# Windowed attention ahead of two MLPs: from 36 slots of four query blocks to 18 slots of eight on 64x64 tiles

## The chip, the cores and the metric

The kernel runs on one core of one Trainium2 chip. The metric is the device time of one execution in microseconds. Three runs of the kernel before took 893.42, 893.79 and 894.28 us, median 893.79.

## What is computed

The input is 4 batches of 8 heads of 576 positions, 64 wide. Each position attends to itself and the 63 before it; the result goes through a gated MLP with RMS norm and through a squared-ReLU MLP. All is fp32.

```python
scores = (q @ k.T) / 8;  mask = (rel >= 0) & (rel < 64)      # rel = query position - key position
scores = where(mask, scores, -1e9);  scores -= scores.max(-1)
attn = exp(scores);  attn = attn / (attn.sum(-1) + 1e-9);  x = attn @ v      # per batch and head
x = x / sqrt(mean(x * x) + 1e-6) * rms_g                      # 2304 tokens x 512
x = (silu(x @ w_gate) * (x @ w_val)) @ w_out                  # d_ff 1536
h = relu(x @ w_in);  out = (h * h) @ w_down                   # d_ff 2048
```

## The kernel before, in words

Channels are on partitions. Two heads of a batch share the 128 partitions, so there are 16 sequences (`SEQS`) of 9 blocks of 64 queries, 144 blocks in all. A block needs the keys of its own 64 positions and of the 64 before. Each of the five engines has its own instruction stream, written out by hand; semaphores join them, and each engine works strictly in the written order.

Attention runs in `GROUPS = 36` groups of four blocks, software-pipelined over slots `g` (0 to 41): in slot g every engine does its part of the group that lags by a constant. TensorE (`slot`, `value_product`) does the scores of group g (L609; 128x128, with the queries of the two heads on the diagonal of a zeroed tile `q_diag`; L604 adds a mask for a sequence's first block), the transposes of group g - 4 (L617, four of `wide`), and in odd slots the value products of two earlier groups (L636, two 128x64 tiles a block). VectorE picks the own keys' columns into place (L1169, `copy_predicated`), takes the maximum (L1178), shifts by it (L1184), and for the group before sums the exponentials (L1175) and inverts (L1181). ScalarE does one Exp per group (L934), copies the transposed weights out of PSUM (L859, `probsT<-bank`) and copies outputs (L859, `acts<-bank`). GpSimd multiplies by the inverse sum (L504) and widens to both key blocks under the mask (L510). Scores, transposes and outputs have two PSUM banks each; banks 0 and 1 are free for the norm.

SP issues all loads in one queue, in the order of the sequences: keys and queries three sequences ahead (a load of keys waits until the sequence whose buffer it takes has its scores), values one ahead (waits on the value products), and between them the first two weight steps (`load_w`) and two chunks of `w_out` (`load_d`).

Tokens are handled in three pairs of 384. The first pair is complete long before the last group, so its squares, norm, splitting into high and low fp32r parts and the first MLP step (`plain(0)`: eight products of six 128x384 matmuls) are spread over slots 16 to 41. Behind the last slot TensorE waits for the last output copy and starts `plain(1)`, then the rest of both MLPs (L661 to L663).

## Time and profile before

| | |
|---|---|
| median of 3 runs | 893.79 us |
| profiled execution | 893.3 us |
| its span, first to last instruction | 891.6 us |
| granted TensorE clock, mean | 1.000 |
| TensorE, VectorE, ScalarE, GpSimd busy | 98%, 63%, 52%, 65% |
| slots of the attention | 0 to 101.7 us |

The profile was taken from one execution. Times are counted from the start of its span. "Busy" is the time between the start and the end of at least one instruction; matmuls overlap, so their mean length (about 0.27 us) says little, and the distance between their starts says more. The fp32 matmuls of the attention show as two MATMUL records each.

### The profile page before, as it was taken

How to read it: one execution, taken by the hardware profiler on the slowest of the kernel's cores; microseconds unless marked ns; L12 is line 12 of the kernel's file. 1: busy time of each engine (PE TensorE's matmuls, PEld its weight loads, DVE VectorE, ACT ScalarE, POOL GpSimd, SP SyncE). 2: the span in 40 equal slices, each digit the busy share in tenths (PEclk: the TensorE clock that was granted, in tenths of full speed). 3: DMA queues.
4: the chain of work that ended last, by engine and by line, in shares of the span. 5: the costliest groups of instructions: out<-in, count | busy, mean ns of one | idle time of the engine just before them, and what ended most of it. 6: DMA issues, size and time to landing. Idle time of an engine off the chain costs nothing.

```text
span 891.6 us, 15074 instructions
## 1 busy us (share of the span) xinstructions
PE 877.7 (98%) x5644; PEld 867.9 (97%) x5644; DVE 561.8 (63%) x735; ACT 463.2 (52%) x800; POOL 575.3 (65%) x539
## 2 busy tenths in 40 slices
PE   7998999999999999999999999999999999999998
PEld 6888999999999999999999999999999999999998
DVE  7778667548657557855556767667377675577222
ACT  3676565644566644455545455554355543455332
POOL 7898479765389757368867368573386653585332
DMA  8996122212222212222221322122422122421122
GB/s 231 263 243 154 53 71 73 71 54 60 79 76 72 68 53 69 73 72 72 71 72 60 82 66 72 54 65 67 148 72 72 54 64 67 148 71 30 49 71 95
DMA packets 105975, 77.00 MB, mean 86 GB/s; under 512 B 24496, under 2 KB 89008, under 8 KB 105904
## 3 DMA queue, kind: packets, MB, share of 16 engines
q1 hardware_dynamic: 105152, 75.60, 30.5%
q8 instruction: 45, 0.74, 0.4%
q10 hardware_dynamic: 752, 0.44, 0.2%
q14 instruction: 26, 0.21, 0.1%
HBM read 71.31 MB, written 4.72 MB: 85 GB/s over the span
## 4 chain that ended last, share of the span: by engine, by line
PE 93%; DMA 3%; DVE 2%; SPq 1%; ACT 0%; issue 0%; POOL 0%; ACTq 0%
PE bank L661 30%; PE bank L662 29%; PE bank L663 29%; DMA q_diag<-in_qT 3%; PE bank L609 2%; PE bank L636 1%; PE bank L617 1%; PE bank L655 0%; PE bank L646 0%; DVE acts L1126 0%; DVE bank L1169 0%; SPq L355 0%; DVE sums L1175 0%; DVE neg_max L1178 0%; DVE probs L1184 0%
## 5 line engine op out<-in xcount | busy, mean ns | idle before, releaser
L661 PE MATMUL bank<-xc_hi,w_hi 128*128 128x384 f32 x844 | 282.8, 335 | 1.7 <-DVE xc_lo L1158 1.0
L663 PE MATMUL bank<-xc_hi,w_lo 128*128 128x384 f32 x844 | 282.0, 334 | 0.0
L662 PE MATMUL bank<-xc_lo,w_hi 128*128 128x384 f32 x844 | 281.9, 334 | 0.0
L552 POOL TENSOR_TENSOR d_lo<-d_raw,d_hi 128x512 fp32r<-128x512 f32 x84 | 127.3, 1516 | 174.5 <-ACT d_hi L859 174.5
L661 PE MATMUL bank<-hs_hi,d_hi 128*128 128x384 f32 x672 | 225.1, 335 | 0.1
L663 PE MATMUL bank<-hs_hi,d_lo 128*128 128x384 f32 x672 | 224.5, 334 | 0.0
L662 PE MATMUL bank<-hs_lo,d_hi 128*128 128x384 f32 x672 | 224.5, 334 | 0.0
L1259 DVE TENSOR_TENSOR hs_lo<-h,hs_hi 128x768 fp32r<-128x768 f32 x84 | 86.4, 1029 | 137.2 <-ACT hs_hi L859 137.0
L661 PEld LDWEIGHTS bank<-xc_hi,w_hi 128*128 128x128 f32 x844 | 158.5, 188 | 2.3 <-DVE xc_lo L1158 1.3
L662 PEld LDWEIGHTS bank<-xc_lo,w_hi 128*128 128x128 f32 x844 | 158.5, 188 | 0.0
L663 PEld LDWEIGHTS bank<-xc_hi,w_lo 128*128 128x128 f32 x844 | 158.4, 188 | 0.0
L859 ACT ACTIVATE hs_hi<-h 128x768 fp32r<-128x768 f32 x84 | 70.9, 843 | 138.7 <-PE bank L663 138.7
L1103 DVE TENSOR_TENSOR w_lo<-w_raw,w_hi 128x1024 fp32r<-128x1024 f32 (+1 forms) x60 | 81.6, 1360 | 82.3 <-ACT w_hi L859 82.2
L661 PEld LDWEIGHTS bank<-hs_hi,d_hi 128*128 128x128 f32 x672 | 126.1, 188 | 1.4 <-issue 0.7
L662 PEld LDWEIGHTS bank<-hs_lo,d_hi 128*128 128x128 f32 x672 | 126.2, 188 | 0.0
L663 PEld LDWEIGHTS bank<-hs_hi,d_lo 128*128 128x128 f32 x672 | 126.2, 188 | 0.0
L859 ACT ACTIVATE w_hi<-w_raw 128x1024 fp32r<-128x1024 f32 (+1 forms) x120 | 111.9, 932 | 0.0
L476 POOL TENSOR_TENSOR w_raw<-w_raw 128x256 f32<-128x256 f32 x58 | 63.7, 1098 | 38.1 <-DMA w_raw<-in_w_val 19.9
L1112 DVE TENSOR_TENSOR w_lo<-w_raw,w_hi 128x768 fp32r<-128x768 f32 (+1 forms) x60 | 72.5, 1209 | 0.0
L545 POOL TENSOR_TENSOR h<-sbb,vb 128x384 f32<-128x384 f32 x34 | 55.7, 1638 | 25.6 <-ACT sbb L983 25.5
L989 ACT ACTIVATE sa<-ga 128x384 f32<-128x384 f32 x58 | 30.5, 526 | 65.9 <-DVE ga L1280 65.8
L859 ACT ACTIVATE c_t<-bank 128x384 f32<-128x384 f32 x58 | 28.5, 492 | 65.3 <-PE bank L663 65.3
(90 smaller groups left out, 1156.0 us busy)
## 6 DMA issues: line engine op xcount, KB each, us to landing
d_raw<-in_w_down SPq DMA_DIRECT2D x48, 256.0 KB, 2.6
w_raw<-in_w_gate SPq DMA_DIRECT2D x36, 256.0 KB, 2.9
w_raw<-in_w_val SPq DMA_DIRECT2D x72, 128.0 KB, 2.9
d_raw<-in_w_out SPq DMA_DIRECT2D x36, 256.0 KB, 2.7
w_raw<-in_w_in SPq DMA_DIRECT2D x24, 256.0 KB, 2.7
w_raw<-in_w_in SPq DMA_DIRECT2D x48, 128.0 KB, 2.6
out_T<-acts SPq DMA_DIRECT2D x24, 192.0 KB, 2.6
k_sb<-in_kT SPq DMA_DIRECT2D x15, 288.0 KB, 4.7
```

The source lines that it names most:

```text
L476: nc.gpsimd.tensor_tensor(raw_part(u, RAW_S3), raw_part(u, RAW_A11), raw_part(u, RAW_A21), ALU.subtract).then_inc(s_add, 1)
L545: nc.gpsimd.tensor_tensor(h_half(n, 1), sbuf_b[:], vb[:], ALU.mult).then_inc(hb_done, 1)
L552: nc.gpsimd.tensor_tensor(d_lo[m % 2][:], d_raw[m % 2][:], d_hi[m % 2][:].bitcast(F32), ALU.subtract).then_inc(dlo_done, 1)
L609: mm = pe.matmul(ps, q_diag[par][:, b, :], keys, start=b > 0, stop=True)
L661: pe.matmul(ps, w_h, v_h, start=first, stop=False, skip_group_check=joined)
L662: pe.matmul(ps, w_h, v_l, start=False, stop=False, skip_group_check=joined)
L663: return pe.matmul(ps, w_l, v_h, start=False, stop=last, skip_group_check=joined)
L859: nc.scalar.activation(to, of, ACT.Copy).then_inc(done, 1)
L989: nc.scalar.activation(sa[:], ga[:], ACT.Silu if first_layer(r) else ACT.Relu).then_inc(act_a_done, 1)
L1103: nc.vector.tensor_tensor(w_lo[u % 2][:, to], w_raw[u % 2][:, of], w_hi[u % 2][:, to].bitcast(F32), ALU.subtract).then_inc(lo1_done, 1)
L1112: nc.vector.tensor_tensor(w_lo[u % 2][:, to], w_raw[u % 2][:, of], w_hi[u % 2][:, to].bitcast(F32), ALU.subtract).then_inc(lo2_done, 1)
L1259: nc.vector.tensor_tensor(hs_lo[m % 2][:], h_chunk(r, m - M0[r]), hs_hi[m % 2][:].bitcast(F32), ALU.subtract).then_inc(hlo_done, 1)
```

## The change

The groups become 18 of eight blocks, four pairs to a group (`UNITS`), in slots 0 to 20. A block's scores are now two 64x64 matmuls, one a head, on four quarters of the array: for blocks 0 to 3 of a group head 0 goes to partitions 0 to 63, for blocks 4 to 7 the heads are crossed. The queries are loaded as they are, without the zeroed tile, the keys in plain order, the values as six blocks per half. Own and previous keys are picked by one mask for all blocks. The maximum is scaled on GpSimd and enters the Exp as its bias; there are eight Exp per group, of 64 columns each, each writing its sum. One transpose takes two blocks. VectorE multiplies the transposed weights by the mask while it takes them out of the single PSUM bank `pt_ps`, once for the own and once for the previous keys; the value products accumulate the two in PSUM. Score banks become two pairs, the outputs share one pair. The norm's banks and slots move (13 to 20), the low halves of the first two weight steps move from VectorE to GpSimd, the order of loads changes.

The diff, cut to what the text speaks of (behind it, `plain(0)` is spread over slots 18 to 20, the squares on ScalarE over slots 7 to 11, `root` in 13, `x_high` in 16 to 20; VectorE normalises in slots 15 to 18 and does `x_low` in 17 to 20):

```diff
 
 SEQS = KT * BATCH
 BLOCKS = SEQS * NBLK
-GU = 4
+UNITS = 4
+GU = 2 * UNITS
 GW = GU * P
 GROUPS = BLOCKS // GU
-S_LAG, N_LAG, T_LAG, PV_LAG, O_LAG = 1, 2, 4, 5, 6
+N_LAG, T_LAG, PV_LAG, O_LAG = 1, 2, 3, 3
 TAIL = GROUPS + O_LAG
-PR = 5
-ER = 3
-QR = 3
+PR = 4
+QR = 4
 VR = 3
 TR = 3
...
+        banks2 = [ctx.enter_context(nc.psum_tensor(f"banks{n}", [P, 1024], F32)) for n in range(4)]
+        bank = [banks2[n // 2][:, n % 2 * 512:(n % 2 + 1) * 512] for n in range(8)]
+        s_ps, pt_ps, o_ps = banks2[0:2], bank[4], banks2[3]
 
...
-                    sp.dma_start(dst[:].rearrange("p m c -> p (m c)"), src[bass.ds(i * P, P), :]).then_inc(v_in[n], 16)
...
+                sp.dma_start(v_sb[n][:].rearrange("p m c -> p (m c)"), v_rows[bass.ds(i * P, P), :]).then_inc(v_in[n], 16)
 
...
             for i in range(SEQS):
+                if i + 1 < SEQS:
+                    load_v(i + 1)
                 if i + QR < SEQS:
                     load_k(i + QR)
                     load_q(i + QR)
-                if i + 1 < SEQS:
-                    load_v(i + 1)
-                if i in (3, 5):
-                    load_w((i - 3) // 2)
-                if i in (8, 9):
-                    load_d(i - 8)
+                if i in (1, 3):
+                    load_w((i - 1) // 2)
+                if i in (9, 10):
+                    load_d(i - 9)
...
+            def low1_plain(u):
+                pool.wait_ge(hi1_done, u + 1)
+                to = slice(0, 3 * HALF_K)
+                nc.gpsimd.tensor_tensor(w_lo[u][:, to], w_raw[u][:, to], w_hi[u][:, to].bitcast(F32),
+                                        ALU.subtract).then_inc(lo1_done, 1)
...
-                    n = g - N_LAG
-                    v = probs[n % PR][:, :, 0:WIN]
+                n = g - N_LAG
+                if 0 <= n < GROUPS:
+                    total = sums[:, n % PR, :]
+                    pool.wait_ge(exp_done, n + 1)
+                    nc.gpsimd.tensor_scalar(total, total, 1e-9, None, ALU.add).then_inc(summed, 1)
+                if g < GROUPS:
+                    peak = neg_max[:, g % PR, :]
+                    pool.wait_ge(maxed, g + 1)
+                    nc.gpsimd.tensor_scalar(peak, peak, SCALE, None, ALU.mult).then_inc(biased, 1)
...
                     pool.wait_ge(inverted, n + 1)
...
+                    nc.gpsimd.tensor_tensor(probs[n % PR][:], probs[n % PR][:],
+                                            by_unit(sums[:, n % PR, :]), ALU.mult).then_inc(scaled, 1)
...
+                if g in (5, 7):
+                    low1_plain((g - 5) // 2)
+                if g in (6, 8):
+                    low2_plain((g - 6) // 2)
+                if g in (9, 10, 11):
+                    add_squares(0, g - 8)
+                if g == 12:
+                    for k in (1, 2, 3):
+                        add_squares(1, k)
+                if g == 14:
...
+            def score(ps, half, seq, b, mask):
+
+                par = seq % QR
+                keys = k_sb[par][:].rearrange("p (n c) -> p n c", c=WIN)
+                for head in range(2):
+                    r = rows(head)
+                    to = ps[rows(head ^ half), :]
+                    if mask:
+                        mm = pe.matmul(to, ident_bf[r, r], first_mask[r, :], start=True, stop=False)
+                    else:
+                        both = keys[r, b - 1:b + 1, :] if b else keys[r, 0:1, :].broadcast_to([WIN, 2, WIN])
+                        mm = pe.matmul(to, q_sb[par][r, b * WIN:(b + 1) * WIN], both, start=b > 0, stop=True)
+                return mm
...
+                        pe.wait_ge(exp_done, g - 1)
+                    for j in range(UNITS):
+                        for half in range(2):
+                            u = half * UNITS + j
+                            seq, b = blocks(g)[u]
+                            ps = s_ps[g % 2][:, u * P:(u + 1) * P]
+                            if b == 0:
+                                score(ps, half, seq, b, True)
+                            mm = score(ps, half, seq, b, False)
...
+                if 0 <= g - PV_LAG < GROUPS:
+                    value_product(g - PV_LAG)
...
+                    pe.wait_ge(scaled, n + 1)
+                    if n >= 1:
+                        pe.wait_ge(pt_out, n)
+                    for j in range(UNITS):
+                        mm = pe.transpose(pt_ps[:, j * P:(j + 1) * P],
+                                          probs[n % PR][:, j, :, :].rearrange("p h c -> p (h c)"), ident[:])
...
+                if n >= 1:
+                    pe.wait_ge(o_out, O_DONE[n])
...
+                for j in range(UNITS):
+                    for own in (1, 0):
+                        for half in range(2):
+                            u = half * UNITS + j
+                            seq, b = blocks(n)[u]
+                            if own or b > 0:
+                                at = (1 - own) * UNITS * P + j * P
+                                v = v_sb[seq % VR][rows(half), held(seq, half).index(b - 1 + own), :]
+                                for head in range(2):
+                                    mm = value(o_ps[rows(head), (UNITS + u) * WIN:(UNITS + u + 1) * WIN],
+                                               v[:, rows(head)],
+                                               probsT[n % TR][rows(half), at:at + P][:, rows(head ^ half)], own, b)
...
+                if g == 17:
+                    pe.wait_ge(exp_done, 17)
+                    spread_half(1, bank[1])
...
+                if g == 13:
+                    token_sums(0, bank[5])
+                if g == 15:
+                    spread_half(0, bank[5])
+                if g == 18:
                     pe.wait_ge(lo1_done, 1)
-                    pe.wait_ge(norm_done, KT)
                     plain(0, "ga", P_A11, "B11")
...
+                    act.wait_ge(biased, g + 1)
+                    if g >= PR:
+                        act.wait_ge(tr_done, g - PR + 1)
+                    for u in range(GU):
+                        mm = nc.scalar.activation(probs[g % PR][:, u % UNITS, u // UNITS, :], s_ps[g % 2][:, u * P:u * P + WIN], ACT.Exp,
+                                                  bias=neg_max[:, g % PR, u:u + 1], scale=SCALE,
+                                                  accum_out=sums[:, g % PR, u:u + 1])
+                    mm.then_inc(exp_done, 1)
...
+                    nc.vector.copy_predicated(
+                        merged, pick[:].unsqueeze(1).broadcast_to([P, GU, WIN]).bitcast(mybir.dt.uint16),
+                        s_view[:, :, 1, :]).then_inc(picked, 1)
                 if g < GROUPS:
+                    if g >= PR:
+                        dve.wait_ge(exp_done, g - PR + 1)
                     dve.wait_ge(picked, g + 1)
-                    nc.vector.tensor_reduce(peak, merged, AX_X, ALU.max, negate=True).then_inc(maxed, 1)
-                if 0 <= g - S_LAG < GROUPS:
-                    dve.wait_ge(summed, g - S_LAG + 1)
-                    nc.vector.reciprocal(total, total).then_inc(inverted, 1)
-                if g < GROUPS:
-                    dve.wait_ge(maxed, g + 1)
-                    nc.vector.tensor_tensor(probs[g % PR][:, :, 0:WIN], merged,
-                                            peak.unsqueeze(2).broadcast_to([P, GU, WIN]), ALU.add).then_inc(shifted, 1)
-
-                if g in (19, 21):
-                    low1((g - 19) // 2)
-                if g in (20, 22):
-                    low2((g - 20) // 2)
-                if g == 28:
-                    mean_square(0, bank[0])
-                if g == 29:
+                    nc.vector.tensor_reduce(neg_max[:, g % PR, :], merged, AX_X, ALU.max,
+                                            negate=True).then_inc(maxed, 1)
+                if 0 <= g - N_LAG < GROUPS:
+                    n = g - N_LAG
+                    dve.wait_ge(summed, n + 1)
+                    nc.vector.reciprocal(sums[:, n % PR, :], sums[:, n % PR, :]).then_inc(inverted, 1)
+                if 0 <= g - T_LAG < GROUPS:
+                    n = g - T_LAG
+                    if n == 0:
+                        dve.wait_ge(consts, CONSTS)
+                    dve.wait_ge(tr_done, n + 1)
+                    if n >= TR:
+                        dve.wait_ge(pv_done, n - TR + 1)
+                    nc.vector.tensor_tensor(
+                        probsT[n % TR][:].rearrange("p (s j q) -> p s j q", s=2, j=UNITS),
+                        pt_ps.rearrange("p (j q) -> p j q", j=UNITS).unsqueeze(1).broadcast_to([P, 2, UNITS, P]),
+                        mask_t[:].rearrange("p s h c -> p s (h c)").unsqueeze(2).broadcast_to([P, 2, UNITS, P]),
+                        ALU.mult).then_inc(pt_out, 1)
```

## Rows read from the trace of the kernel before

**Rows 1.** The page: busy time and share of each engine.

```profile
PE 877.7 (98%) x5644; PEld 867.9 (97%) x5644; DVE 561.8 (63%) x735; ACT 463.2 (52%) x800; POOL 575.3 (65%) x539
```

**Rows 2.** Busy time by engine and stretch, then granted clock, DMA, GB/s.

```profile
12.00:72.00 60.00, 57.67 (x746) 52.31 (x747) 44.66 (x141) 38.84 (x98) 53.38 (x61) 1.00 1.12 256
72.00:101.70 29.70, 26.74 (x318) 24.34 (x316) 22.60 (x48) 19.49 (x44) 24.44 (x25) 1.00 0.36 101
101.70:891.60 789.90, 786.71 (x4548) 785.09 (x4548) 486.72 (x527) 402.75 (x657) 490.42 (x426) 1.00 0.24 71
```

**Rows 3.** Chain that ended last at the hand-over (start, length, what).

```profile
101.12 0.39 ACT acts L859
...
101.77 0.41 PE bank L661
102.18 0.17 PE bank L662
```

**Rows 4.** Timeline of TensorE, one pair of groups (start, length first).

```profile
24.46 1.16 PE L609 MATMUL bank<-k_sb,q_diag 128*128 128x128 f32 x8
25.46 0.60 PE L617 MATMUL bank<-ident,wide 128*128 128x128 f32 x4
...
27.43 0.34 PE L636 MATMUL bank<-probsT,v_even 128*64 128x64 f32 x4
27.59 0.29 PE L636 MATMUL bank<-probsT,v_odd 128*64 128x64 f32 x4
...
28.74 0.38 PE L609 MATMUL bank<-k_sb,q_diag 128*128 128x128 f32 x1
```

**Rows 5.** DMA issues, 12 to 72 us: KB each, us to landing.

```profile
q_diag<-in_qT SPq DMA_DIRECT2D x24, 144.0 KB, 6.4
```

**Rows 6.** Waits before 130 us: total, times, longest.

```profile
DVE bank L1169 <- PE bank L609: 16.2, 16, 2.4
...
PE bank L604 <- DMA q_diag<-in_qT: 6.5, 4, 4.8
```

**Rows 7.** VectorE, groups by line before 130 us (busy, mean ns).

```profile
L1169 DVE COPY_PREDICATED bank<-valid,bank 128x256 f32<-128x256 uint16 x36 | 15.3, 425 | 16.5 <-PE bank L609 16.2
...
L1178 DVE TENSOR_REDUCE neg_max<-bank 128x4 f32<-128x256 f32 x36 | 14.9, 414 | 0.0
L1181 DVE RECIPROCAL sums<-sums 128x4 f32<-128x4 f32 x36 | 6.0, 167 | 0.0
...
L1103 DVE TENSOR_TENSOR w_lo<-w_raw,w_hi 128x1024 fp32r<-128x1024 f32 x4 | 4.9, 1225 | 5.2 <-ACT w_hi L859 5.2
```

**Rows 8.** ScalarE, groups by line before 130 us.

```profile
L859 ACT ACTIVATE probsT<-bank 128x512 f32<-128x512 f32 x36 | 21.3, 592 | 12.1 <-PE bank L617 12.0
L934 ACT ACTIVATE probs<-probs 128x256 f32<-128x256 f32 x36 | 15.0, 417 | 23.5 <-DVE probs L1184 23.2
L859 ACT ACTIVATE acts<-bank 128x256 f32<-128x256 f32 x24 | 8.9, 369 | 1.8 <-PE bank L636 1.8
...
L888 ACT ACTIVATE sq<-acts 128x384 f32<-128x384 f32 x8 | 4.1, 517 | 0.1
...
L934 ACT ACT_TABLE_LOAD x2 | 2.6, 1283 | 2.6 <-issue 2.6
...
L859 ACT ACTIVATE acts<-bank 128x64 f32<-128x64 f32 x8 | 1.7, 211 | 0.0
```

**Rows 9.** Timeline of ScalarE, two output copies of 128 columns.

```profile
27.56 0.42 ACT L859 ACTIVATE acts<-bank 128x128 f32<-128x128 f32 x2
```

**Rows 10.** GpSimd, groups by line before 130 us.

```profile
L510 POOL TENSOR_TENSOR wide<-probs,valid 128x512 f32<-128x512 f32 x36 | 42.9, 1191 | 5.0
L504 POOL TENSOR_TENSOR probs<-probs,sums 128x256 f32<-128x256 f32 x36 | 22.8, 633 | 7.3 <-DVE sums L1181 7.2
...
L466 POOL MEMSET probs<- 128x4 f32 x5 | 0.2, 112 | 0.0
```

**Rows 11.** Timeline of TensorE, the first score passes.

```profile
4.84 4.33 PE L609 MATMUL bank<-k_sb,q_diag 128*128 128x128 f32 x18
```

332 lines of the change are left out of this document (136 added, 196 removed).

## The prediction

> **What bounds the kernel now.** I read the profile page first [rows 1]: TensorE is busy for 98% of the span, no other engine for more than 65%. Then a table of three stretches [rows 2]. The change touches only what lies before 101.7 us. From there to the end TensorE is busy for 786.7 of 789.9 us on code that the change leaves alone, so whatever is won or lost is the moment at which this stretch starts: the matmuls of the second plain step, which now follow the last output copy at 101.77 us [rows 3]. I call that moment H. The profiled execution took 893.3 us, of which 891.6 are its span; the time after is 893.3 - 101.8 + H. (The median of the runs is 893.8, 0.5 above the profiled one; 0.2% of it, 1.8 us, is about what a measurement of this kernel can tell from no change.)
>
> Then the order of work on TensorE in one pair of attention groups [rows 4]: scores from 24.46, transposes from 25.46, again scores and transposes, values from 27.43, and the next scores at 28.74. That is 4.28 us for eight blocks, without a gap, and 18 such pairs make 77 us. The reader should see that every fp32 matmul is two passes: 8 score passes and the change of tile shape behind the values in 1.00 us (0.11 us a pass), 4 transposes in 0.43, 32 value passes in 1.31. Value passes are cheap because two 128x64 tiles run side by side: 4 passes (two matmuls) start every 0.12 us, 29 ns each. The transfers are the second bound: over 12 to 72 us the 16 DMA engines are busy beyond 100% at 256 GB/s [rows 2], with the query tiles landing after 6.4 us in 144 KB pieces of 256-byte runs [rows 5]. TensorE still waited only 6.5 us for them, most of it at the start, and VectorE waited 16.2 us for score matmuls [rows 6], so it has room.
>
> **The change part by part, for one slot of eight blocks.**
>
> *Scores.* The zero-padded query tile goes, and 8 products of 128x128 become 16 of 64x64, 32 passes of 128 columns on four quarter tiles. The trace has no quarter tile. Bounds for a pass: 58 ns if a tile's own cadence (0.12 us for its two passes, [rows 4]) is never overlapped; 15 ns if four tiles overlap as two do now. I take 22, near the low end, because the value passes show that neighbours with different output partitions overlap fully. 32 x 0.022 = 0.70, plus 0.17 for the change of tile shape (the last transpose starts at about 27.23, values at 27.43, against 0.11 within a row of transposes).
>
> *Values.* The 16 matmuls of 64 columns over 128 keys become 32 over 64 keys, less the two that a first block lacks: 60 passes on average. Bounds 15 and 58 ns again; I take 25, since two tiles manage 29 today. 60 x 0.025 = 1.50. This is more than the 1.31 of now.
>
> *Transposes.* 4 in place of 8: 0.44, plus 0.17 for the shape. TensorE then works 0.87 + 1.50 + 0.61 = 3.0 us per slot against 4.28.
>
> *VectorE.* It loses the sum (0.42) and the shift (like 0.42) per four blocks and gains the masked product. From 256 elements in 0.425 and 1024 in 1.225 [rows 7], an element costs 1.04 ns: predicated copy of 512 elements 0.69, maximum 0.68, reciprocal 0.17, product of 1024 elements out of PSUM 1.22. Together 2.8, off the path as a sum.
>
> *ScalarE.* It loses two copies of 0.592 and two Exp of 0.417 [rows 8] and gains eight Exp of 64 columns with a bias from memory and a sum written out. Lower bound 0.09: two 128-column copies take 0.42, so the second adds 0.15, less 0.06 for 64 columns fewer [rows 8, 9]. Upper bound 0.42, the whole Exp of 256 columns. I take 0.33: the 0.21 of a lone 64-column copy plus 0.12 for delivering the sum, as an operation this small cannot cost less than what a second copy adds. 8 x 0.33 + 0.7 for the two output copies = 3.3. Here the Trainium skill bears on one term: "ScalarE: Activation LUTs", section "What ACT_TABLE_LOAD costs", has 280 + 0.833 N ns for a bias from memory and 93 ns of overlap, an estimate of 0.24 for each without the sum; ScalarE would then need 2.6 us a slot and never be late, and H would be some 2 us earlier. No row of this trace shows a bias from memory.
>
> *GpSimd.* Its widening (1.191) and scaling (0.633) per four blocks become one scaling of 512 elements, 1.2 by the row of the widening, and two operations on eight numbers, 0.11 each [rows 10]. 1.4 a slot, so it has room for the low halves of the first two weight steps moved there from VectorE (two of 768 and two of 256 elements, 1.8 and 0.6 each by the widening row) and for the adds.
>
> *DMA.* Queries come as one 288 KB piece like the keys, values as 384 KB in place of 512: 0.98 MB per pair of heads instead of 1.11. At today's 256 GB/s that is 3.8 us per nine blocks, 3.4 a slot, and less if whole rows move faster than 256-byte runs. The first two weight steps and chunks are issued two pairs of heads earlier or one later, each behind the same queue; 1 MB of weights is 4 us of transfer before slot 8, covered while loads run two slots ahead. The value load waits for the product three groups on, and key and query loads queue behind it on SP; they then have some 4.7 us until their slot. I allow 1 us.
>
> *The cycle that sets a slot.* One bank for the transposed tiles closes a ring between two engines: transposes 0.60 from first start to last end, product 1.22, values 1.50, shape 0.17, two hand-overs of 0.05. That is 3.6 us; scores (0.87) fit beside the product. ScalarE's 3.3 lies just under it. So T = 3.6 against 4.28.
>
> *Start and normalisation.* First scores at 4.8 as now. At the start a pass takes twice as long: 18 in 4.33 us, 0.24 each, against 0.111 later [rows 11, 4], though the granted clock reads 1.00 there. Slot 1 needs the second query load, issued only after the first landed: 4.6 + 3.4 = 8.0 (the first loads take 4.0 from their issue to the first score). With half-rate scores and the fill of the ring, slot 3 starts at about 13. Fifteen slots to slot 18: 54 us. Squares (8 x 0.517), the high parts of the weights (two each of 768 and 256 elements, about 0.8 and 0.4) and two table loads (1.283 each) [rows 8] are 9 us on ScalarE, whose slack is 0.3 a slot, 4 in all: +5. In front of slot 17 TensorE waits for the Exp of group 16, so that 1.6 to 3 us, which overlapped before, lie open: +3 with the spread. Slot 18 begins at 75. The tail holds three value groups (4.5), two sets of transposes (1.2), the eight products of the first plain step, six matmuls of 0.18 each [rows 3], 8.6 in all, and 4.5 of waits for products, normalised halves and the last output copy: 18.8. H = 93.8.
>
> **Time: 893.3 - 101.8 + 93.8 = 885.3 us.** Nothing behind H changes: the sums of the third weight step on GpSimd, due about 9 us after H, start with a load issued 15 us before H.
>
> **The rivals.**
> *Quarter tiles overlap fully and Exp is cheap.* Passes of 15 ns and Exp of 0.24 or less: the ring is 3.0, the transfers hold it at about 3.2. Twelve of the 0.4 x 15 saved plus a shorter tail give H near 82: 873.5. For it: two tiles overlap perfectly today. Against: 2 instructions every 15 ns has no row.
> *The Exp with its sum sets the slot (slower).* Place: ScalarE, eight instructions per slot where one or two stood. It decides from 0.38 each on; at 0.42 a slot is 8 x 0.42 + 0.7 + the extra 0.6 = 4.7, H = 106: 897.5. At 0.38 the result is a draw. For it: per-instruction cost, not columns, dominates at 64 columns (0.21 against 0.37 for 256).
> *TensorE falls to half its rate.* Its busy share drops from 96% [rows 2] to some 80% with an idle stretch in each slot while the product runs. Passes twice as long give 5.7 a slot: H near 117, 908.5. Rows 11 show the half rate only behind an idle start, and short waits later never brought it back. The Trainium skill's "TensorE: Matmul & The Clock Gate", section "A second HAM failure mode: psum-queue depth-cycling", names exactly such idling between groups as a cause of falling back from 2.4 to 1.2 GHz; the trace of before neither confirms nor excludes it.
> *Quarter tiles do not overlap.* 58 ns a pass: ring 6.4, H near 140, 931. The change then doesn't do what it says.
>
> **How the numbers follow.** Forecast 885.3 (own range 878 to 893): 0.50. Cheap case: 0.17. A draw with Exp near 0.38: 0.07. Slower by Exp: 0.13. Half rate: 0.08. No overlap: 0.05. Faster 0.49 + 0.16 = 0.65, same 0.09, slower 0.26. For 8 in 10 the range leaves out half rate, no overlap and the far end of the cheap case: 872 to 900.
>
> **What would show it.** The time between score groups should be 3.6 us; value passes 25 ns apart; Exp starts 0.33 apart; the product waiting for transposes and the values for the product in turn; the stretch behind H unchanged at 789.9 us. I am wrong on the ring if TensorE waits for Exp instead; on the quarter tiles if four passes of different tiles start farther than 0.12 us apart; on the clock if the same pass has two lengths in the middle of the attention.

## The result and the profile after

| | before | after |
|---|---|---|
| median | 894.03 us (4 runs, 893.42 to 898.21) | 885.12 us (4 runs, 884.67 to 885.68) |
| ratio after/before, 95% interval | | 0.9891 [0.9860, 0.9921] |
| profiled execution, its span | 893.3, 891.6 | 885.7, 884.0 |
| H, start of the second plain step's matmuls | 101.8 | 94.2 |
| behind H | 789.9 | 789.8 |

The kernel is 1.1% faster, and all of it lies ahead of H. The page of the changed kernel, first its busy times, then TensorE's granted clock in 40 slices (tenths), then the queue of its instruction packets (packets, MB, share of 16 engines):

```profile
PE 858.6 (97%) x6388; PEld 846.9 (96%) x6388; DVE 548.2 (62%) x617; ACT 472.3 (53%) x1000; POOL 543.9 (62%) x517
...
PEclk9998999999999999999999999999999999999999
...
q8 instruction: 51, 0.84, 0.4%
```

TensorE is busy for 19 us less than in [rows 1], in 744 instructions more, yet the span is only 7.6 us shorter: TensorE now stands still for longer ahead of H. Where, is in the busy times by stretch. The stretches are those of the argument: first slots, slots 3 to 6, slots 7 to 12, slots 13 to 16, slot 17 and the tail, and what lies behind H. The columns are busy us (instructions) of TensorE, its weight loads, VectorE, ScalarE, GpSimd, then granted clock, DMA share and GB/s.

```profile
4.80:14.65 9.85, 7.22 (x106) 5.78 (x107) 3.94 (x7) 4.94 (x32) 1.84 (x5) 1.00 0.89 314
14.65:31.80 17.15, 12.75 (x395) 11.18 (x395) 12.31 (x19) 14.28 (x82) 9.46 (x17) 1.00 0.72 222
31.80:52.30 20.50, 17.44 (x594) 14.24 (x594) 14.76 (x23) 19.48 (x107) 13.87 (x23) 1.00 0.87 279
52.30:74.50 22.20, 16.64 (x420) 14.39 (x419) 13.92 (x23) 19.61 (x96) 11.82 (x19) 0.88 0.50 165
74.50:94.20 19.70, 17.84 (x337) 16.31 (x337) 15.98 (x19) 10.03 (x30) 11.65 (x12) 0.88 0.28 76
94.20:884.00 789.80, 786.67 (x4550) 785.01 (x4548) 487.32 (x528) 402.66 (x656) 491.93 (x426) 1.00 0.25 71
```

The last line answers to the last of [rows 2]: 789.8 against 789.9, the same work. In the third line ScalarE is busy for 19.48 of 20.50 us. These are six slots of 3.42 us on average (one by one 2.6, 3.1, 3.6, 4.0, 4.1 and 3.1), and ScalarE is the fullest engine in them; whether it sets them is what the experiments ask. One slot there, first on TensorE, then ScalarE's first Exps of it (start, length, engine, what, count; [idle time <- released by]):

```profile
34.38 1.10 PE L613 MATMUL banks<-k_sb,q_sb 64*64 64x128 f32 x32
35.77 1.15 PE L669 MATMUL banks<-probsT,v_sb 64*64 64x64 f32 x60 [0.28 <-DVE probsT L1224]
36.85 0.66 PE L643 MATMUL banks<-ident,probs 128*128 128x128 f32 x4
```

```profile
34.84 0.31 ACT L976 ACTIVATE probs<-banks,neg_max 128x64 f32<-128x64 f32 x1 [0.24 <-POOL neg_max L519]
35.05 0.19 ACT L976 ACTIVATION_READ_ACCUMULATOR probs<-banks,neg_max 128x1 f32 x1
35.14 0.30 ACT L976 ACTIVATE probs<-banks,neg_max 128x64 f32<-128x64 f32 x1
...
35.43 0.31 ACT L976 ACTIVATE probs<-banks,neg_max 128x64 f32<-128x64 f32 x1
```

An Exp that also writes its sum is two instructions, and the next one starts 0.29 us behind it (34.84, 35.14, 35.43). The 60 value passes, of 1.15 us from first start to last end, start within 0.93 us, 16 ns apart. The groups by line before H (busy us, mean ns | idle us before, releaser) answer to [rows 7, 8, 10]:

```profile
L976 ACT ACTIVATE probs<-banks,neg_max 128x64 f32<-128x64 f32 x144 | 43.1, 344 | 10.2 <-POOL neg_max L519 10.0
L976 ACT ACTIVATION_READ_ACCUMULATOR probs<-banks,neg_max 128x1 f32 x144 | 33.8, 238 | 0.0
...
L1224 DVE TENSOR_TENSOR probsT<-banks,mask_t 128x1024 f32<-128x1024 f32 x18 | 21.6, 1203 | 4.1 <-PE banks L643 4.0
...
L522 POOL TENSOR_TENSOR probs<-probs,sums 128x512 f32<-128x512 f32 x18 | 19.0, 1058 | 1.0 <-DVE sums L1216 1.0
...
L1211 DVE TENSOR_REDUCE neg_max<-banks 128x8 f32<-128x512 f32 x18 | 12.5, 692 | 1.6
L1204 DVE COPY_PREDICATED banks<-pick,banks 128x512 f32<-128x512 uint16 x18 | 12.4, 690 | 20.4 <-PE banks L613 20.4
...
L515 POOL TENSOR_SCALAR sums<-sums 128x8 f32<-128x8 f32 x18 | 4.3, 237 | 21.7 <-ACT probs L976 21.5
```

TensorE's idle time in the two stretches with the lower granted clock (slots 14 and 17):

```profile
56.71 1.50 PE L677 MATMUL banks<-ones,sq 128*128 128x1 f32 x12 [1.00 <-POOL sq L507]
...
59.36 2.07 PE L669 MATMUL banks<-probsT,v_sb 64*64 64x64 f32 x60
...
72.90 1.65 PE L684 MATMUL banks<-sq,ones 128*128 128x128 f32 x6 [3.53 <-ACT probs L976]
74.48 1.99 PE L613 MATMUL banks<-k_sb,q_sb 64*64 64x128 f32 x32
76.24 1.93 PE L669 MATMUL banks<-probsT,v_sb 64*64 64x64 f32 x60
```

The same 32 score passes take 1.99 us here and 1.10 in the slot above, the same 60 value passes 1.93 to 2.07 and 1.15: the same pass has two lengths. The longer one is that of the lower clock level, 1.2 GHz: the granted clock reads 0.50 from 74.5 to 79.2 us, and 0.72 over 72 to 84 us, part at one level and part at the other. In front of each of the two stretches stands a wait of TensorE, of 1.00 and of 3.53 us.

The start of each slot's scores, read off the timelines of this kernel and of those below, is the measure for the rest. The mask products are counted out, and every profile is shifted so that its first matmul stands at 4.84 us as in the changed kernel (by 0.21 us at most; the lines of views are not shifted):

| kernel | slot 3 | 7 | 13 | 14 | 15 | 16 | 17 | H | median us | ratio to before |
|---|---|---|---|---|---|---|---|---|---|---|
| changed | 14.7 | 31.8 | 52.3 | 58.1 | 62.3 | 66.2 | 74.5 | 94.2 | 885.12 | 0.9891 [0.9860, 0.9921] |
| changed, again | 14.6 | 31.2 | 51.9 | 57.8 | 60.4 | 65.7 | 73.2 | 92.4 | 884.39 | 0.9886 [0.9868, 0.9904] |
| no sum | 13.8 | 30.6 | 51.0 | 56.7 | 60.7 | 64.6 | 70.8 | 90.0 | 880.51 | 0.9838 [0.9825, 0.9850] |
| two banks | 14.6 | 31.2 | 51.4 | 57.7 | 60.2 | 65.5 | 73.0 | 91.2 | 888.49 | 0.9922 [0.9897, 0.9947] |
| copies on VectorE | 14.7 | 30.2 | 51.0 | 57.2 | 61.5 | 65.7 | 73.2 | 94.0 | 886.26 | 0.9908 [0.9893, 0.9922] |
| spread in bank 5 | 14.7 | 30.3 | 51.7 | 57.6 | 61.8 | 65.9 | 73.7 | 93.7 | 885.15 | 0.9892 [0.9879, 0.9905] |
| spread behind slot 17 | 14.6 | 31.5 | 52.8 | 58.7 | 62.9 | 67.0 | 70.0 | 89.8 | 880.25 | 0.9834 [0.9816, 0.9852] |
| keys ahead of values | 14.6 | 30.6 | 54.1 | 59.9 | 64.1 | 68.2 | 76.6 | 96.5 | 886.09 | 0.9905 [0.9888, 0.9923] |
| both orders | 14.7 | 28.5 | 52.6 | 58.5 | 62.7 | 66.6 | 69.8 | 89.7 | 881.22 | 0.9839 [0.9821, 0.9858] |
| one half at a time | 16.0 | 34.1 | 62.1 | 67.7 | 72.9 | 77.3 | 84.9 | 109.3 | 892.08 | 0.9981 [0.9961, 1.0000] |
| small loads | 14.6 | 28.0 | 48.7 | 55.0 | 59.8 | 63.7 | 71.2 | 90.8 | 881.50 | 0.9854 [0.9842, 0.9867] |
| token sums behind scores | 14.6 | 30.7 | 51.4 | 55.5 | 60.6 | 65.2 | 68.1 | 87.7 | 878.93 | 0.9826 [0.9813, 0.9839] |
| and early copies on VectorE | 14.6 | 30.6 | 51.9 | 55.1 | 61.3 | 65.8 | 69.0 | 88.8 | 881.53 | 0.9864 [0.9843, 0.9884] |

The kernels ran in three series, on more than one chip, with the kernel before at 895.15, 894.78 and 894.86 us beside them; small differences are read from the ratios, and where their intervals overlap, a difference is not clear of noise. A profile is one execution; between two executions of one kernel slots 4 to 12 shift by up to some 2 us.

### The profile page after: what moved, and what is told of

It reads as the page before. It is cut to its first block, busy times and chain, and to the rows that moved or that the text cites. A ratio compares the mean times of both kernels' runs of the same rounds, so it can differ in the third digit from the quotient of the medians.

```text
span 884.0 us, 16543 instructions
## 1 busy us (share of the span) xinstructions
PE 858.6 (97%) x6388; PEld 846.9 (96%) x6388; DVE 548.2 (62%) x617; ACT 472.3 (53%) x1000; POOL 543.9 (62%) x517
## 4 chain that ended last, share of the span: by engine, by line
PE 93%; ACT 2%; DVE 2%; DMA 1%; issue 1%; POOL 1%; SPq 0%; DVEq 0%; POOLq 0%
PE banks L703 30%; PE banks L705 30%; PE banks L704 30%; ACT probs L976 2%; PE banks L613 1%; PE banks L669 1%; DMA q_sb<-in_qT 1%; DVE probsT L1224 1%; PE banks L684 0%; PE banks L677 0%; PE banks L643 0%; POOL sq L507 0%; DVE neg_max L1211 0%; DVE banks L1204 0%; DVE acts L1164 0%
## 5 line engine op out<-in xcount | busy, mean ns | idle before, releaser
L703 PE MATMUL banks<-xc_hi,w_hi 128*128 128x384 f32 x844 | 282.5, 335 | 0.2 <-DVE xc_lo L1196 0.2
L705 PE MATMUL banks<-xc_hi,w_lo 128*128 128x384 f32 x844 | 281.9, 334 | 0.0
L704 PE MATMUL banks<-xc_lo,w_hi 128*128 128x384 f32 x844 | 281.9, 334 | 0.0
L703 PE MATMUL banks<-hs_hi,d_hi 128*128 128x384 f32 x672 | 225.1, 335 | 0.1
L705 PE MATMUL banks<-hs_hi,d_lo 128*128 128x384 f32 x672 | 224.5, 334 | 0.0
L704 PE MATMUL banks<-hs_lo,d_hi 128*128 128x384 f32 x672 | 224.5, 334 | 0.0
L703 PEld LDWEIGHTS banks<-xc_hi,w_hi 128*128 128x128 f32 x844 | 158.5, 188 | 0.5 <-DVE xc_lo L1196 0.5
L704 PEld LDWEIGHTS banks<-xc_lo,w_hi 128*128 128x128 f32 x844 | 158.5, 188 | 0.0
L705 PEld LDWEIGHTS banks<-xc_hi,w_lo 128*128 128x128 f32 x844 | 158.4, 188 | 0.0
L899 ACT ACTIVATE hs_hi<-h 128x768 fp32r<-128x768 f32 x84 | 70.8, 843 | 138.7 <-PE banks L705 138.7
L704 PEld LDWEIGHTS banks<-hs_lo,d_hi 128*128 128x128 f32 x672 | 126.2, 188 | 0.0
L1030 ACT ACTIVATE sa<-ga 128x384 f32<-128x384 f32 x58 | 30.5, 526 | 65.9 <-DVE ga L1323 65.8
L899 ACT ACTIVATE c_t<-banks 128x384 f32<-128x384 f32 x58 | 28.5, 492 | 65.3 <-PE banks L705 65.3
```

What stands on the lines that cost most here:

```text
L703: pe.matmul(ps, w_h, v_h, start=first, stop=False, skip_group_check=joined)
L704: pe.matmul(ps, w_h, v_l, start=False, stop=False, skip_group_check=joined)
L705: return pe.matmul(ps, w_l, v_h, start=False, stop=last, skip_group_check=joined)
L899: nc.scalar.activation(to, of, ACT.Copy).then_inc(done, 1)
L1030: nc.scalar.activation(sa[:], ga[:], ACT.Silu if first_layer(r) else ACT.Relu).then_inc(act_a_done, 1)
```

## The experiments

The first four part two theories. A: ScalarE with its eight Exps a slot holds the attention. B: the ring transposes, product, values through one bank of transposed tiles holds it.

**No sum.**

```diff
                     for u in range(GU):
                         mm = nc.scalar.activation(probs[...], s_ps[g % 2][...], ACT.Exp,
-                                                  bias=neg_max[:, g % PR, u:u + 1], scale=SCALE,
-                                                  accum_out=sums[:, g % PR, u:u + 1])
+                                                  bias=neg_max[:, g % PR, u:u + 1], scale=SCALE)
```

> The changed kernel without the sum that each Exp writes out (the sums stay at one, so the weights are not normalised; this part is left out). In the changed kernel an Exp and its accumulator read start 0.29 us apart, 0.09 of it behind the read: 144 x 0.09 = 13 us of ScalarE. Theory A (ScalarE sets the slot in the middle of the attention, it is busy 19.5 of 20.5 us there): 4 to 9 us faster than the changed kernel's 885.1. Theory B (the ring transposes, product, values sets it, as predicted): within 1.5 us of it.

Measured 880.51 us, ratio 0.9838, 4.6 us under the 885.12 that the expectation starts from: theory A's range. ScalarE's eight Exps of a slot, in its timeline:

```profile
51.82 1.81 ACT L977 ACTIVATE probs<-banks,neg_max 128x64 f32<-128x64 f32 x8
```

1.81 us against the 2.48 of the changed kernel: 0.21 from start to start in place of 0.29. But slots 7 to 12 still take 3.4 us each (30.6 to 51.0), though ScalarE is no longer full there:

```profile
31.80:52.30 20.50, 17.41 (x596) 14.13 (x590) 15.88 (x25) 17.20 (x66) 14.57 (x25) 1.00 0.87 289
```

Of these six slots four take 3.05 to 3.15 us and two, starting at 39.9 and 43.9, take 4.0; in those two TensorE's values have a gap of 0.96 and 0.98 us in their midst, which the profile puts down to "issue". So where ScalarE has room a slot without a gap takes the ring's 3.05 to 3.15 us, and 2 us are lost to the gaps. The changed kernel has two such long slots too, and slots of 3.1 beside them, so this run alone doesn't say that ScalarE held its middle; the kernel with small loads, below, does. What the lighter Exp won came mostly outside the middle: slots 0 to 2 (0.9 us) and from slot 13 on (51.0 to 90.0, 39.0 us against 40.5 and 41.9 in the two profiles of the changed kernel).

**Two banks for the transposed tiles.**

```diff
-        s_ps, pt_ps, o_ps = banks2[0:2], bank[4], banks2[3]
+        s_ps, o_ps = banks2[0:2], banks2[3]
+        def pt_bank(n):
+            return bank[4 + (n % 2 if n <= 10 else 0)]
...
-                if 0 <= g - PV_LAG < GROUPS:
-                    value_product(g - PV_LAG)
                 if 0 <= g - T_LAG < GROUPS:
                     n = g - T_LAG
+                    pt_ps = pt_bank(n)
                     pe.wait_ge(scaled, n + 1)
-                    if n >= 1:
-                        pe.wait_ge(pt_out, n)
+                    if n >= 2:
+                        pe.wait_ge(pt_out, n - 1 if n <= 10 else n)
...
+                if 0 <= g - PV_LAG < GROUPS:
+                    value_product(g - PV_LAG)
```

> The changed kernel with two PSUM banks for the transposed tiles up to group 10 and the transposes ahead of the values in a slot, so that the product runs beside the values and the ring is open. Theory B: the slot falls from 3.6 towards the 3.1 us of ScalarE in nine slots, 4 to 6 us faster. Theory A: within 1.5 us of 885.1, because ScalarE's work is unchanged.

Measured 888.49 us, between 882.8 and 892.1 in six runs. Neither theory had it slower, and its ratio of 0.9922 [0.9897, 0.9947] overlaps with that of the changed kernel. The 4 to 6 us of theory B are not there: in the profiled execution, the fastest of the six, slots 7 to 12 take 3.37 us each against 3.42. As a limit in slots 3 to 10 the ring falls. Why the other five runs are 4 to 9 us longer, no profile shows; it stays open. Their mean granted clock is 0.992 to 0.996, like that of the changed kernel's runs, and that of the profiled one is 1.000: it ran ahead of H without any stretch at 1.2 GHz, though it has the same wait ahead of the second spread:

```profile
72.29 0.94 PE L688 MATMUL banks<-sq,ones 128*128 128x128 f32 x6 [3.47 <-ACT probs L980]
73.16 1.10 PE L616 MATMUL banks<-k_sb,q_sb 64*64 64x128 f32 x32
```

So a wait of this length doesn't by itself bring the lower clock.

**The output copies on VectorE.**

```diff
 # ScalarE
-                    act.wait_ge(pv_done, n + 1)
-                    for run in runs_of(n):
-                        to, of = output(n, run)
-                        copy(to, of, o_out)
 # VectorE, ahead of the reciprocal
+                    dve.wait_ge(pv_done, n + 1)
+                    for run in runs_of(n):
+                        to, of = output(n, run)
+                        nc.vector.tensor_copy(to, of).then_inc(o_out, 1)
```

> The changed kernel with the output copies (0.7 us a slot) on VectorE in front of the reciprocal, off ScalarE. Theory A: ScalarE has 2.3 us of Exp left a slot, 5 to 9 us faster than 885.1, until VectorE (2.8 + 0.7 = 3.5 a slot) holds it. Theory B: the copies push the product back within the ring, no change to 6 us slower.

Measured 886.26 us, ratio 0.9908: theory A's gain is not there. Busy time over slots 7 to 12, and what TensorE and ScalarE waited for from 24 to 50 us (us in total, times, longest):

```profile
31.80:52.30 20.50, 16.53 (x555) 13.38 (x547) 18.60 (x34) 17.55 (x99) 14.18 (x22) 1.00 0.85 275
```

```profile
ACT probs L970 <- POOL neg_max L519: 4.2, 6, 1.3
PE banks L669 <- DVE probsT L1224: 2.8, 5, 0.9
```

ScalarE went from 19.5 to 17.6 us and VectorE from 14.8 to 18.6: ScalarE now waits for the maximum that VectorE makes later. Over its own slots 7 to 12, 3.47 us each, VectorE is busy for 3.0 us a slot, ScalarE for 3.0, and the ring takes 3.0: none is full. The load moved and nothing was won; that the engines now wait for each other in turn is argued from these waits, not shown.

**The second spread in bank 5.**

```diff
-                if g == 17:
-                    pe.wait_ge(exp_done, 17)
-                    spread_half(1, bank[1])
                 slot(g)
+                if g == 16:
+                    pe.wait_ge(norm_done, KT)
+                    spread_half(1, bank[5])
...
-                        normalise(half_cols(0, k, 1), k, bank[1][:, 0:NT])
+                        normalise(half_cols(0, k, 1), k, bank[5][:, 0:NT])
```

> The changed kernel with the second half's spread in bank 5 at the end of slot 16 instead of bank 1 ahead of slot 17, so that TensorE no longer waits there for the Exp of group 16 (3.5 us idle, after which passes start at twice the distance until 79.2 us). If the idle stretch brings the half rate (1.2 in place of 2.4 GHz), both go: 4 to 6 us faster than 885.1, and score passes of slot 17 in 0.83 us rather than 1.57. If the half rate comes from something else, 1 to 3 us faster and 1.57 stays.

Measured 885.15 us, no gain. The wait kept its place and changed its name; one line of TensorE's timeline:

```profile
72.27 1.65 PE L684 MATMUL banks<-sq,ones 128*128 128x128 f32 x6 [2.96 <-DVE acts L1165]
```

The normalising products that free bank 5 stand behind the maximum and the product of slot 16 on VectorE and end at 72.2, where the Exps of group 16, for which the changed kernel waits, end at 72.9. It is no test of the idle time, since the idle time stayed. The test is the next one.

The second series has theories S (an engine held up by the order of its own program) and T (the stream behind is full and takes back what is won). The changed kernel ran along:

> The changed kernel, nothing edited, beside the three that follow, so that they can be compared with it on one chip. Both theories: 885 us within 1 us, the second plain step starting at 94.2 us; the waits of 1.5 and 1.8 us for q_sb ahead of slots 5 to 7 and the 3.8 us without a TensorE instruction ahead of the second spread at 69.1 to 72.9 us come back.

884.39 us; H was 92.4 in its profile. It came within 1 us; the wait for q_sb was one of 3.1 us ahead of slot 6 in place of two, 2.9 us together, ahead of slots 6 and 7, and the one ahead of the second spread came back as it was. New is a stretch at the lower clock level in slot 6, behind the wait of 3.1 us; granted clock and DMA share are the first two figures behind the last bracket:

```profile
28.00:32.00 4.00, 4.00 (x106) 3.55 (x100) 2.25 (x4) 1.81 (x12) 1.78 (x4) 0.60 0.66 180
```

**The second spread behind slot 17.**

```diff
+                slot(g)
                 if g == 17:
                     pe.wait_ge(exp_done, 17)
                     spread_half(1, bank[1])
-                slot(g)
```

> One thing is moved: TensorE issues the second spread behind the whole of slot 17 instead of ahead of it, so that the scores of group 17 no longer stand behind its wait for the Exps of group 16. Everything is computed. Theory S (an engine held up by the order of its own program): slot 17's scores start at 69.4 us and not 74.5, the Exps of group 17 end 4 us earlier, and the second plain step starts at about 90.2: 881 us, 4 us under the changed kernel. Theory T (the stream behind is full, so that what is won at one place is lost at the next, as it was with the copies on VectorE and with the spread in bank 5): within 1 us of the changed kernel, with the idle time of TensorE found again ahead of the values of groups 15 and 16.

Measured 880.25 us, 4.1 under the changed kernel of the series, and the intervals of the ratios don't meet: theory S. TensorE's timeline from slot 17 on, and the granted clock of two stretches (the figure behind the last bracket):

```profile
70.04 1.10 PE L613 MATMUL banks<-k_sb,q_sb 64*64 64x128 f32 x32
72.02 1.15 PE L669 MATMUL banks<-probsT,v_sb 64*64 64x64 f32 x60 [0.87 <-DVE probsT L1224]
...
73.64 0.94 PE L684 MATMUL banks<-sq,ones 128*128 128x128 f32 x6
```

```profile
72.00:84.00 12.00, 9.89 (x220) 8.81 (x221) 11.90 (x17) 10.41 (x40) 7.81 (x12) 1.00 0.43 125
84.00:89.80 5.80, 5.80 (x92) 5.48 (x91) 4.79 (x5) 2.10 (x4) 3.42 (x3) 1.00 0.01 3
```

The scores of group 17 needed nothing that the spread waits for, and now stand at 70.0 instead of 73.2 to 74.5. The longest wait is 1.1 us, the passes have their short length, and the clock reads 1.00 where it read 0.72 to 0.86. From 84 us to H TensorE has no free time left.

**Keys and queries ahead of values in SyncE's loop, and both orders together.**

```diff
             for i in range(SEQS):
-                if i + 1 < SEQS:
-                    load_v(i + 1)
                 if i + QR < SEQS:
                     load_k(i + QR)
                     load_q(i + QR)
+                if i + 1 < SEQS:
+                    load_v(i + 1)
```

> SyncE's loop issues the loads of keys and queries four sequences ahead first and the load of values behind them; before, the load of values and its wait for the value product stood ahead. Everything is computed. Theory S: the 3.3 us that TensorE waited for q_sb at 26 to 32 us go, and because ScalarE was busy for 14.3 of the 17.1 us of slots 3 to 6, at most 2.8 us are won: 1.5 to 2.8 us, 882.5 to 883.5 us. Theory T: ScalarE, with 2.3 us of Exps and 0.7 us of copies a slot and 1.8 us roundings of weights in slots 4 and 6, takes the place of the load, and less than 0.7 us is left.

> The spread behind slot 17 and the loads of keys ahead of those of values, together. Everything is computed. Theory S: the two lie at different places of one chain and add up, 5.5 to 6.8 us under the changed kernel, 878.5 to 880 us. Theory T: within 1.5 us of it.

Measured 886.09 and 881.22 us: the load order wins nothing, alone (1.7 above the changed kernel) or with the spread (1.0 above the kernel with the spread alone). Theory T had less than 0.7 won and none lost; by the ratios, whose intervals overlap, the loss isn't clear of noise. TensorE's waits from 24 to 50 us, first of the changed kernel as it ran again, then of this one:

```profile
PE banks L613 <- DMA q_sb<-in_qT: 3.1, 1, 3.1
...
PE banks L669 <- issue: 1.1, 2, 0.6
```

```profile
PE banks L669 <- issue: 3.5, 3, 1.7
...
PE banks L613 <- issue: 1.0, 2, 0.5
PE banks L669 <- DMA v_sb<-in_v_rows: 0.8, 1, 0.8
```

The wait for queries went, as meant. In its place came one for values, 0.8, and 3.5 us of gaps inside the groups of values, for which the profile has no releaser; its clock also reads 0.50 at 26 to 28 and at 50 to 52 us. With both orders slots 3 to 6 take 13.8 us in place of 16.6, but slot 9 alone takes 6.8, with a single gap of 2.8 us in its scores and the lower clock behind it, and slot 13 stands at 52.6.

**One half at a time.**

```diff
-                for j in range(UNITS):
-                    for own in (1, 0):
-                        for half in range(2):
+                for half in range(2):
+                    for j in range(UNITS):
+                        for own in (1, 0):
...
-                    for j in range(UNITS):
-                        for half in range(2):
+                    for half in range(2):
+                        for j in range(UNITS):
```

> The loops of the scores and of the value product run over one half of the rows first and then over the other, so that neighbouring matmuls alternate between two 64x64 tiles (scores) and two (values) and not among four; the number of matmuls and what they compute are the same. Theory Q (passes on different quarters overlap, which is why the 60 value matmuls took 0.94 us from first to last, 16 ns each, and not the 1.50 us of the forecast): they take 1.3 to 1.9 us, the 32 scores 0.83 to 1.3, and the kernel is 1 to 6 us slower than the changed one. Rival I (a pass of 64 columns costs 16 ns wherever it runs): 0.93 and 0.83 us again, the time within 1 us.

Measured 892.08 us, 7 us above the changed kernel: theory Q, by 1 us more than its range. One slot at a granted clock of 1.00 on TensorE:

```profile
45.91 1.54 PE L613 MATMUL banks<-k_sb,q_sb 64*64 64x128 f32 x32
47.22 1.80 PE L669 MATMUL banks<-probsT,v_sb 64*64 64x64 f32 x60
```

The same 60 passes start within 1.58 us and not 0.93 (27 ns each, not 16), the 32 score passes within 1.27 and not 0.83 (41 ns, not 27). So a pass is that cheap when its neighbours use all four quarters. (The new order also brings the two value products that add up in one place of PSUM closer together; but the score products, which add to nothing but a mask, slow down as well.) The profiled execution was the longest of twelve (891.2 to 900.8 us, its span 899.0), hence its H of 109.3; its granted clock was 0.75 over 31.8 to 52.3 us, so part of what it is longer than the others is the half rate. The mean clock of the other runs, 0.989 to 0.996, is near that of the changed kernel (0.990 to 0.998), so the half rate explains little of the median's 7 us.

**Small loads.**

```diff
-                sp.dma_start(k_sb[par][:], kT[bass.ds(i * P, P), :]).then_inc(qk_in[par], 16)
+                w = slice(0, SEQ if i < QR else WIN)
+                sp.dma_start(k_sb[par][:, w], kT[bass.ds(i * P, P), w]).then_inc(qk_in[par], 16)
 # queries likewise; values from sequence VR on 128 columns of 768
```

> The loads of keys and queries from the fifth sequence on bring only the first 64 of their columns, the loads of values from the fourth on only 128 of theirs; the rest of those buffers keeps what the earlier sequences left, so part of the attention is computed on other data. All waits and all instructions stay. Theory F (the gaps of 0.5 to 1.7 us inside the groups of small matmuls are TensorE's instructions arriving late, because their packets of 16 KB share the 16 DMA engines with the loads): the waits for q_sb and nearly all gaps of over 0.4 us inside a group of values go, slots 4 to 12 take 3.3 to 3.6 us each and not 4.0, and the kernel is 3 to 6 us under the changed one. Rival S (ScalarE holds the stream): gaps and waits go, but slot 13 starts no more than 1.5 us earlier and the kernel is within 1.5 us.

Measured 881.50 us, ratio 0.9854: 2.9 us under the changed kernel as it ran again, 3.6 under its first median. TensorE's waits from 24 to 50 us, and slots 7 to 12:

```profile
PE banks L672 <- DVE probsT L1227: 3.3, 7, 0.8
```

```profile
31.80:52.30 20.50, 16.44 (x574) 13.37 (x563) 15.27 (x23) 20.50 (x116) 16.04 (x24) 1.00 0.19 47
```

The time is at the lower end of theory F's range, and slots 4 to 12 take 3.4 us each, as it said; rival S, with 1.5 us at most, is out as a forecast of the time. The gaps inside the values are all gone with the transfers (DMA share 0.19 and not 0.87), as theory F said: "issue" is no longer among TensorE's matmul waits of this stretch. But slots 7 to 12 take 3.45 us each (28.0 to 48.7), no less than the 3.42 of the changed kernel, because ScalarE is busy for 20.50 of 20.50 us (and for all of its own slots 7 to 12, 28.0 to 48.7): with the gaps gone ScalarE sets these slots, and in that stretch the gaps had cost next to nothing, as rival S said. What the transfers cost lies in slots 3 to 6, which take 13.4 us against 16.6 in the changed kernel's second profile; the 3.2 us are all still there at slot 13 (48.7 for 51.9), and half of them at H (90.8 for 92.4).

The last two build on the kernel with the spread moved.

**Token sums behind the scores of slot 14.**

```diff
                     mm.then_inc(qk_done, 1)
+                if g == 14:
+                    token_sums(0, bank[5])
                 if 0 <= g - PV_LAG < GROUPS:
...
-                if g == 13:
-                    token_sums(0, bank[5])
 # VectorE
                     nc.vector.tensor_reduce(neg_max...).then_inc(maxed, 1)
+                if g == 14:
+                    mean_square(0, bank[5])
...
-                if g == 13:
-                    mean_square(0, bank[5])
```

> On top of the spread behind slot 17, the token sums (12 matmuls of one column, and the wait of about 1.3 us ahead of them) stand behind the scores of slot 14 and not ahead of them, and VectorE's reading of them behind its maximum of slot 14. Everything is computed. Theory S: the scores of slot 14 start 2.8 us earlier and at full rate, the Exps of slot 14 about 2 us earlier, and all behind them: 1 to 2.5 us under the kernel with the spread moved, 878 to 879.3 us. Rival T: ScalarE, which had 10.8 us of work in the 12 us there, holds it: within 0.7 us of it.

Measured 878.93 us, 1.3 under the kernel with the spread moved by the medians, which is in theory S's range, but 0.7 by the ratios (0.9826 and 0.9834), whose intervals overlap; the two ran in different series. So the gain is not clear of noise. TensorE around slot 14:

```profile
55.58 0.82 PE L613 MATMUL banks<-k_sb,q_sb 64*64 64x128 f32 x22
56.34 1.50 PE L679 MATMUL banks<-ones,sq 128*128 128x1 f32 x12
57.76 1.16 PE L671 MATMUL banks<-probsT,v_sb 64*64 64x64 f32 x60
```

The scores of slot 14 start 3.2 us earlier (55.5 for 58.7), and H is 2.1 us earlier. But slot 13, ahead of anything that the edit touches, is 1.4 us earlier already, so of the profiles' difference not all is the edit's.

**And the copies of groups 0 to 9 on VectorE.**

The edit is that of the copies above, for the first ten groups only.

> The former kernel, with the copies of the outputs of groups 0 to 9 on VectorE and not on ScalarE (0.7 us of 3.1 us of ScalarE's work a slot; VectorE then has 3.6 us a slot in the middle). Everything is computed. Theory S, ScalarE as the holder of slots 7 to 12: 1 to 2.5 us under the former kernel. Rival T: VectorE takes its place, within 0.7 us.

Measured 881.53 us (879.3 to 885.3), 2.6 above the former kernel: neither, though nearer to theory T. From 31 to 51 us ScalarE is busy for 16.6 us and VectorE for 16.8, against 19.3 and 14.8 in the former kernel, so neither is full, and the clock reads 0.91 there, against 1.00. What made it slower is not shown.

The fastest kernel by its median is thus the changed one with two waits of TensorE moved behind matmuls that don't need them: 878.93 us, ratio 0.9826 [0.9813, 0.9839] to the kernel before, 0.7% under the changed one.

## Why the prediction came out as it did

The forecast was 885.3 us, the median is 885.12. Its sum was H; of the parts of H, two were off in opposite ways.

| part of H | forecast | measured |
|---|---|---|
| start of slot 3 | 13 | 14.7 |
| slots 3 to 6 | 4 x 3.6 | 17.1 |
| slots 7 to 12 | 6 x 3.6 | 20.5 |
| slots 13 to 17 on TensorE | 5 x 3.6, and 8 of allowances | 26.9 (to 79.2) |
| slot 18 begins | 75 | 79.2 |
| tail | 18.8 | 15.0 |
| H | 93.8 | 94.2 |

*Value passes: mis-sized.* 25 ns was taken from two tiles of 128x64 side by side; four quarters in turn gave 16 ns, 0.93 us and not 1.50. Kept to two quarters at a time, the same passes cost 27 ns: the forecast's 25 fitted two tiles, and the order of the loops in the change uses four. The tail had three such groups, 1.7 us too much. Its waits of 4.5 us were 1.9 in fact (1.32 and 0.33 for products, 0.21 for a half of x), 2.6 too much; the rest of it was 0.5 longer. Together that is the tail's 3.8. The rival of full overlap and a cheap Exp, at 15 ns a pass, was right on the value passes, though not on the score passes, and its H near 82 did not come, because ScalarE and the transfers stood just behind. (Its sum can't be followed: 0.4 x 15 is 6 us, and it takes off twelve.)

*Score passes.* Forecast 22 ns, measured 27 (0.83 for 32); with the shape change 0.9 to 1.0 us a group, as forecast within 0.1.

*Transposes, VectorE, GpSimd.* 0.66 from first start to last end for 0.60; copy 0.69, maximum 0.69, reciprocal 0.20, product 1.20 for 0.69, 0.68, 0.17, 1.22; scaling 1.06 for 1.2. The operation on eight numbers on GpSimd is 0.24, twice the forecast, taken from a memset of four numbers; it lies between maximum and Exp, but ScalarE waited for it only 0.2 us in slots 7 to 12; 6.4 of the 10.0 us that it waited there in all were one wait in the first slots.

*Exp with bias and sum: 0.33 forecast, 0.29 measured.* The bounds held it. The rival in which ScalarE sets the slot happened, at less than the price that it needed to end slower: eight Exps and the copies are 3.0 us, with the squares and the roundings of the weights 3.25 a slot in slots 7 to 12. The forecast's sign for being wrong on the ring, TensorE waiting for Exp, hardly shows (in the small-loads kernel two waits, 0.6 us); it was the busy time of ScalarE that told. The Trainium skill's "ScalarE: Activation LUTs", section "What ACT_TABLE_LOAD costs", gave an estimate of 0.24 without the sum. The trace of the kernel without the sum agrees roughly, with 0.21; the sum's 0.08 on top is in the traces alone.

*The ring: right as a mechanism, wrong as the limit.* With the measured 0.94 for the values it is 0.60 + 1.22 + 0.94 + 0.17 + 0.10 = 3.03 us, and the undisturbed slots of the kernel without sums took 3.05 to 3.15. The forecast had it at 3.6 because of the value passes, and ScalarE under it; measured, ScalarE (3.25 of work, slots of 3.4) is above the ring. The sum hardly noticed, because the slots came out at 3.42, near 3.6, for another reason than the forecast's; that is luck.

*Transfers: the step that failed.* "I allow 1 us", says the forecast of the loads of keys and queries that queue behind the load of values, and even this 1 us is not among the terms that give H: the sum has the loads at nothing. Slots 3 to 6 took 2.7 us more than forecast, and the kernel with small loads has them 3.2 us shorter than the changed one's second profile (about 1.0 of this is the low clock in slot 6 there: values 1.75 for 1.16 us, transposes 1.11 for 0.66). It is the largest single error of the sum. The row behind it is in the chain of waits of the changed kernel (start, length, what):

```profile
26.49 5.25 DMA q_sb<-in_qT
31.78 0.94 PE banks L613 x25
```

Q's load was issued at 26.49, behind the one of values at 25.65, and landed 5.25 us later, while the DMA share was 0.96 (24 to 32 us). TensorE had stood still for 1.54 us by then, so it needed the load 3.8 us after its issue, where the forecast had 4.7. That simply issuing it sooner would mend it was my next belief, and fell too: the kernel with keys ahead of values was no faster.

*Start.* Slot 3 came 1.65 us late; the first Exps of eight, with scores at twice their later length ahead of them (32 passes in 2.00 us and not 1.10, though the granted clock reads 1.00 there), hold slot 2 until 11.50 us. Without sums it started 0.9 us earlier, so half of this is the price of the Exp, which the forecast had not counted in the fill.

*The half rate.* The rival of a fall to half rate, as it stood, did not happen: no kernel runs all of its middle at 0.50. What happened is short stretches, two in the first profile of the changed kernel, behind waits of 1.00 and 3.53 us, and two in the second, in slots 6 and 17. By its own sign, the same pass with two lengths in the middle of the attention, the forecast was wrong on the clock. Twelve of the thirteen profiles have such a stretch somewhere. A wait of TensorE stands ahead of most of them, but the wait does not decide: slot 17 has the long wait and the fall in eight profiles and the wait alone in the one of two banks, slot 14 of the changed kernel has its wait of 1.0 us with the fall in one profile and without in the other, and in the kernel with early copies on VectorE a wait of 0.45 us came with it. In the four kernels with the spread moved the clock is 1.00 from 64 us to H. The Trainium skill's "TensorE: Matmul & The Clock Gate", section "A second HAM failure mode: psum-queue depth-cycling", has frequent short idling between groups of matmuls as what makes the clock swing between its two levels. The traces agree in part: idling stands ahead of the falls and the long fall went with its wait, but here single waits stand there, and the same wait is found without a fall. The half rate of slot 14 cost little: the run without it was 1.6 us faster through slot 14 and then waited 1.27 us ahead of slot 16, where the difference was 0.5.

*The allowance of 3 us in front of slot 17* was too small: slots 16 and 17 took 13.0 us on TensorE (66.2 to 79.2) and not 7.2, with 3.5 us of wait, the spread and the half rate in them. The 5 us for ScalarE's other work made up for it, as slots 13 to 15 took only 3.1 us over 3 x 3.6. Moving the spread won 4.1: what I had not seen is that most of it need not be paid, as the scores behind the spread don't depend on it.

*Behind H:* 789.8 for 789.9.

So the forecast's centre is partly luck: 4.2 us late at slot 18 (1.65 start, 2.7 transfers, 0.9 in slots 13 to 17, less 1.1 in slots 7 to 12), 3.8 early in the tail.

## What to carry to other kernels

Look at what stands behind each wait in the order of an engine's program and ask whether it needs what the wait is for: one such move won 4.1 us here and a second one up to 1.3 more, not clear of noise, while moving load from the fullest engine to another won nothing, as the engines then waited for each other. Price a tile shape by the order in which its neighbours come, not by its size: the same matmuls cost 16 or 27 ns a pass. Where several loads share one queue with a wait in front, count the time from issue to need against landings under load (5.25 us), and expect that an earlier issue pushes on something else.
